# A blockwise delta-rule attention: the inverse is spread by VectorE, its rows are placed whole, and the block gather moves one chunk ahead

## The reference

```python
k_n = k / (np.linalg.norm(k, axis=-1, keepdims=True) + 1e-06)
for t in range(S):
    y[:, :, t] = einsum('bhd,bhde->bhe', q[:, :, t], state)
    v_old = einsum('bhde,bhd->bhe', state, k_n[:, :, t])
    state = state + beta_t * einsum('bhd,bhe->bhde', k_n[:, :, t], v_t - v_old)
```

## Time and profile before

| What | Value |
|---|---|
| Median of 3 runs | 909.26 us (906.07 to 910.19) |
| The profiled execution, its own time | 906.9 us |
| Its span, first to last instruction | 905.0 us |
| PE matmul busy | 808.8 us (89%) |
| DVE busy | 510.0 us (56%) |
| ACT busy | 340.2 us (38%) |
| POOL busy | 163.8 us (18%) |
| End of PE's last attention product | 313.58 us |
| First operation of `dense` on DVE | 317.95 us |

### The profile page before, as it was taken

The page is one execution under the profiler, slowest core; times in us unless marked ns, Lnnn a source line. Parts: engine busy times, 40 slices in busy tenths (PEclk is TensorE's granted clock), DMA queues, the critical chain, the costliest instruction groups (busy, mean ns, idle before and its releaser), DMA issues.

```text
span 905.0 us, 24872 instructions
## 1 busy us (share of the span) xinstructions
PE 808.8 (89%) x10976; PEld 571.8 (63%) x10976; DVE 510.0 (56%) x1212; ACT 340.2 (38%) x659; POOL 163.8 (18%) x195
## 2 busy tenths in 40 slices
PE   5487777888877689999999999999999999999998
PEld 4487777788877635566566656665656666666664
DVE  5666656676665157554336333636454776767522
ACT  3365555555554314322222122414233343433311
POOL 6131323132120001030003001001221332323200
PEclk9998999888999879999999999999999999999999
DMA  8022432231110022301000100000000000000001
GB/s 192 18 74 72 122 73 57 73 74 56 55 39 21 30 74 92 105 1 36 18 27 27 53 1 27 27 1 1 1 1 1 1 19 18 27 18 27 28 27 53
DMA packets 45048, 37.70 MB, mean 42 GB/s; under 512 B 27401, under 2 KB 39052, under 8 KB 44940
## 3 DMA queue, kind: packets, MB, share of 16 engines
q1 hardware_dynamic: 38020, 30.95, 12.3%
q10 hardware_dynamic: 6920, 5.15, 2.0%
HBM read 26.65 MB, written 4.72 MB: 35 GB/s over the span
## 4 chain that ended last, share of the span: by engine, by line
PE 80%; issue 8%; DVE 6%; ACT 4%; DMA 1%; SPq 1%; POOL 0%; DVEq 0%; ACTq 0%
PE bank L298 16%; PE bank L1033 5%; PE bank L1081 5%; PE bank L1079 5%; PE bank L1035 5%; PE bank L1080 5%; PE bank L1034 5%; PE bank L1017 3%; PE bank L1019 3%; PE bank L1018 3%; PE bank L330 3%; PE bank L967 2%; PE bank L353 2%; DVE hT_lo L1451 2%; PE bank L973 2%
## 5 line engine op out<-in xcount | busy, mean ns | idle before, releaser
L1199 ACT ACTIVATE hT_hi<-bank 128x384 f16<-128x384 f32 x96 | 46.8, 489 | 160.9 <-PE bank L1019 160.8
L1033 PE MATMUL bank<-wA,hT_hi 128*128 128x384 f16 x288 | 94.0, 326 | 2.8 <-DVE hT_lo L1451 2.8
L1451 DVE SCALAR_TENSOR_TENSOR hT_lo<-bank,hT_hi 128x384 f16<-128x384 f32 x96 | 53.2, 555 | 73.6 <-ACT hT_hi L1199 73.4
L1017 PE MATMUL bank<-unT,wA 128*128 128x384 f16 x288 | 93.9, 326 | 0.3 <-DVE hT_lo L1451 0.3
L1019 PE MATMUL bank<-unT,wA 128*128 128x384 f16 x288 | 93.9, 326 | 0.0
L1018 PE MATMUL bank<-unT,wA 128*128 128x384 f16 x288 | 93.9, 326 | 0.0
L1035 PE MATMUL bank<-wA,hT_lo 128*128 128x384 f16 x288 | 93.9, 326 | 0.0
L1034 PE MATMUL bank<-wA,hT_hi 128*128 128x384 f16 x288 | 93.9, 326 | 0.0
L298 PE MATMUL bank<-TT,AP 64*64 64x64 f32 x768 | 40.4, 281 | 55.3 <-issue 55.3
L298 PE MATMUL bank<-Yv,ET 64*64 64x48 f32 x2304 | 74.3, 218 | 4.6 <-ACT Yv L436 2.4
L298 PEld LDWEIGHTS bank<-Yv,ET 64*64 64x64 f32 x2304 | 72.1, 135 | 7.2 <-ACT Yv L436 4.6
(11 more groups left out here) (200 smaller groups left out, 1703.8 us busy)
## 6 DMA issues: line engine op xcount, KB each, us to landing
Kb<-k_dram SPq DMA_DIRECT2D x24, 192.0 KB, 3.4
Vv<-v_dram SPq DMA_DIRECT2D x12, 384.0 KB, 3.4
z_first<-w_dram SPq DMA_DIRECT2D x8, 576.0 KB, 3.9
z_first<-wt_dram SPq DMA_DIRECT2D x8, 576.0 KB, 3.7
out_dram<-hT_hi SPq DMA_DIRECT2D x24, 192.0 KB, 1.8
KQ<-q_dram SPq DMA_DIRECT2D x44, 96.0 KB, 2.3
X<-Yo ACTq DMA_DIRECT2D x12, 192.0 KB
X<-Yo ACTq DMA_DIRECT2D x10, 189.0 KB
```

What stands on the lines that cost most here:

```text
L1017: pe.matmul(out, w1[0][:, k, cols], unT[0][:, k, :], start=(k == 0), stop=False)
L1033: pe.matmul(out, hT[0][:, f, cols], w2[0][:, f, :], start=(f == 0), stop=False)
L1199: act.activation(hT[0][:, f, :], bank[3 + m % 3][:, 0:TG * P], ACT.Relu).then_inc(s_hh, 1)
L1451: dve.scalar_tensor_tensor(hT[1][:, f, :], bank[3 + m % 3][:, 0:TG * P], 0.0, hT[0][:, f, :], ALU.max, ALU.subtract).then_inc(s_hl, 1)
```

## The change

1. **Spread by DVE.** `scaled_u` no longer writes Us. Two `scalar_tensor_tensor` operations multiply the inverse by a row mask and by beta over the norm, and write both halves of Ux. ACT's `spread`, the tensor Us and the semaphore `s_sp` are gone.
2. **Layout.** Dy is now [P, BLK, NG, 2] instead of [P, BLK, 2, NG], and To is [P, NG, 2, BLK] instead of [P, BLK, 2, NG]. So the gather (ACT's and DVE's half) writes every second element, the transpose in `blocks_out` writes in steps of 16 elements, and `placed` reads rows of 32 contiguous elements instead of elements 32 apart. The row masks move with it, so that the choice of halves into Rb becomes one addition of two slices instead of two masked operations; IN falls from 6 to 5.
3. **Order on DVE.** `make_x` comes ahead of both `mask_e`; `blocks_out(c + 1)` follows `scaled_u(c + 1)` at once, ahead of `norm` or `scale`; and `blocks_in` is called for c+2 at the end of the turn instead of for c+1 before the elimination.
4. **Order on PE.** `predicted(c)` comes ahead of both corners, `grow(c)` ahead of both `direct`.
5. **Order on ACT.** `placed(c + 1)` comes right after `grown(c)`, ahead of both `output` copies, and `root` after them.

The block of SP is untouched by the diff: every load waits on the same count of the same semaphore as before.

```diff
@@ attention, tensors
-        Dy = sb("Dy", [P, BLK, 2, NG])
+        Dy = sb("Dy", [P, BLK, NG, 2])
-        To = sb("To", [P, BLK, 2, NG])
+        To = sb("To", [P, NG, 2, BLK])
-        Us = sb("Us", [P, BLK, BLK])
@@ PE, turn c
             for c in range(C0, NC):
+                predicted(c)
                 corner(c, 0)
-                predicted(c)
                 corner(c, 1)
...
                 out = queried(c)
+                grow(c)
                 direct(c, 0, out)
-                grow(c)
                 direct(c, 1, out)
@@ ACT
-                    copy(Dy[:, :, x, :], Ab[:, n % RA, :, BLK * x:BLK * (x + 1)].rearrange("p g j -> p j g"),
-                         scale=rows[:, 5:6]).then_inc(s_hb, 1)
-            def spread(n):
-                act.wait_ge(s_us, n + 1)
-                for x in range(2):
-                    copy(Ux[:, :, x, :], Us[:], scale=rows[:, 3 + x:4 + x]).then_inc(s_sp, 1)
+                    copy(Dy[:, :, :, x], Ab[:, n % RA, :, BLK * x:BLK * (x + 1)].rearrange("p g j -> p j g"),
+                         scale=rows[:, 5 + x:6 + x]).then_inc(s_hb, 1)
...
-                    copy(TT[:, :, 2 * BLK * y:2 * BLK * (y + 1)].rearrange("p g (x i) -> p g x i", x=2),
-                         To[:].rearrange("p i x g -> p g x i"), scale=rows[:, 5 + y:6 + y]).then_inc(s_tt, 1)
+                    copy(TT[:, :, 2 * BLK * y:2 * BLK * (y + 1)], To[:].rearrange("p g x i -> p g (x i)"),
+                         scale=rows[:, 9 + y:10 + y]).then_inc(s_tt, 1)
@@ ACT, turn c
                 copied_y(c, 3)
+                grown(c)
+                placed(c + 1)
+                output(c, 0)
+                output(c, 1)
                 if c % 2:
                     root((c + 3) // 2)
-                grown(c)
-                spread(c + 1)
-                output(c, 0)
-                placed(c + 1)
-                output(c, 1)
                 store(c)
@@ DVE, blocks_in, scaled_u, blocks_out
-                dve.tensor_scalar(Rb[:], Tt[:, :, 0, :], rows[:, 3:4], None, ALU.mult).then_inc(s_in, 1)
+                dve.tensor_tensor(Rb[:], Tt[:, :, 0, :], Tt[:, :, 1, :], ALU.add).then_inc(s_in, 1)
                 dve.wait_ge(s_in, at + 4)
-                dve.scalar_tensor_tensor(Rb[:], Tt[:, :, 1, :], rows[:, 4:5], Rb[:], ALU.mult, ALU.add).then_inc(s_in, 1)
+                dve.tensor_tensor(Ti[:], Rb[:], by, ALU.mult).then_inc(s_in, 1)
                 dve.wait_ge(s_in, at + 5)
-                dve.tensor_tensor(Ti[:], Rb[:], by, ALU.mult).then_inc(s_in, 1)
-                dve.wait_ge(s_in, at + 6)
...
-                dve.tensor_tensor(Us[:].rearrange("p i k -> p k i"), U[:], by, ALU.mult).then_inc(s_us, 1)
+                for x in range(2):
+                    dve.scalar_tensor_tensor(Ux[:, :, x, :].rearrange("p i k -> p k i"), U[:], rows[:, 3 + x:4 + x], by, ALU.mult,
+                                             ALU.mult).then_inc(s_us, 1)
...
-                dve.transpose(To[:].rearrange("p i x g -> p (i x g)"), Ux[:].rearrange("p i x k -> p (i x k)")).then_inc(s_to, 1)
+                dve.transpose(To[:].rearrange("p g x i -> p i (g x)"), Ux[:].rearrange("p i x k -> p (i x k)")).then_inc(s_to, 1)
@@ DVE, turn c
             for c in range(C0, NC):
+                make_x(c)
                 mask_e(c, 0)
-                make_x(c)
                 mask_e(c, 1)
-                blocks_in(c + 1)
-                eliminate(c + 1, (1, 2, 3, 4, 5, 6, 7))
-                if c < 0 and c % 2 == 0:
-                    scale((c + 2) // 2)
-                eliminate(c + 1, (8, 9, 10, 11, 12, 13, 14))
+                eliminate(c + 1, (1, 2, 3, 4, 5, 6, 7, 8, 9, 10, 11, 12, 13, 14))
                 scaled_u(c + 1)
+                blocks_out(c + 1)
                 if c % 2:
                     norm((c + 3) // 2)
-                elif c >= 0:
+                else:
                     scale((c + 2) // 2)
-                blocks_out(c + 1)
+                blocks_in(c + 2)
```

More of the change, by code:

```diff
@@ L68, in constants @@
     mU = np.broadcast_to(upper.reshape(1, BLK * BLK), (P, BLK * BLK))
-    z = (p // BLK) % 4
-    rows = np.concatenate([t[:, None] // BLK == np.arange(3)[None, :], z[:, None] % 2 == np.arange(2)[None, :],
-                           z[:, None] // 2 == np.arange(2)[None, :]], 1)
+    x, y, odd = (p // BLK) % 2, (p // (2 * BLK)) % 2, p % 2
+    rows = np.concatenate([t[:, None] // BLK == np.arange(3)[None, :], odd[:, None] == np.arange(2)[None, :],
+                           (2 * y + x)[:, None] == np.arange(4)[None, :], y[:, None] == np.arange(2)[None, :]], 1)
     return {
@@ L116, in attention @@
         mU = sb("mU", [P, BLK * BLK])
-        rows = sb("rows", [P, 7])
+        rows = sb("rows", [P, 11])
         bt = sb("bt", [P, NC * NG])
@@ L120, in attention @@
         ms = sb("ms", [P, 2, 2 * NG])
-        cd = sb("cd", [P, 2, 2, NG])
+        cd = sb("cd", [P, 2, NG, 2])
         cx = sb("cx", [P, 2, 2, BLK])
@@ L135, in attention @@
         s_in, s_iv = sem("block_steps"), sem("inverse_steps")
[L136 to L137 removed]
+        s_hb, s_us, s_to, s_tt = sem("upper_blocks"), sem("inverse_scaled"), sem("inverse_turned"), sem("TT_made")
         s_e, s_et = sem("E_product"), sem("E_masked")
@@ L204, in attention @@
         STEPS = 2 + 28
-        IN = 6
+        IN = 5
         NS = 11
@@ L574, in scale @@
                 if pair >= 2:
-                    dve.wait_ge(s_us, 2 * pair - 2)
+                    dve.wait_ge(s_us, 2 * (2 * pair - 2))
                 m = ms[:, pair % 2, :]
-                both = [P, 2, 2, NG]
+                both = [P, 2, NG, 2]
                 steps = [
@@ L586, in scale @@
                     lambda: dve.tensor_tensor(
-                        cd[:], nr[:, 5, :].rearrange("p (n g) -> p n g", n=2).unsqueeze(2).broadcast_to(both),
-                        bt[:, 2 * pair * NG:2 * (pair + 1) * NG].rearrange("p (n g) -> p n g", n=2).unsqueeze(2).broadcast_to(both),
+                        cd[:], nr[:, 5, :].rearrange("p (n g) -> p n g", n=2).unsqueeze(3).broadcast_to(both),
+                        bt[:, 2 * pair * NG:2 * (pair + 1) * NG].rearrange("p (n g) -> p n g", n=2).unsqueeze(3).broadcast_to(both),
                         ALU.mult),
-                    lambda: dve.transpose(cx[:].rearrange("p n x i -> p (n x i)"), cd[:].rearrange("p n x g -> p (n x g)")),
+                    lambda: dve.transpose(cx[:].rearrange("p n x i -> p (n x i)"), cd[:].rearrange("p n g x -> p (n g x)")),
                     lambda: dve.tensor_scalar(cT[:, pair % 2], cx[:, :, 0, :], rows[:, 3:4], None, ALU.mult),
@@ L605, in blocks_in @@
                     dve.wait_ge(s_hb, 2 * n + x + 1)
-                    dve.scalar_tensor_tensor(Dy[:, :, x, :],
+                    dve.scalar_tensor_tensor(Dy[:, :, :, x],
                                              Ab[:, n % RA, :, BLK * (x + 2):BLK * (x + 3)].rearrange("p g j -> p j g"),
-                                             rows[:, 6:7], Dy[:, :, x, :], ALU.mult, ALU.add).then_inc(s_in, 1)
+                                             rows[:, 7 + x:8 + x], Dy[:, :, :, x], ALU.mult, ALU.add).then_inc(s_in, 1)
                 dve.wait_ge(s_in, at + 2)
-                dve.transpose(Tt[:].rearrange("p j x i -> p (j x i)"), Dy[:].rearrange("p j x g -> p (j x g)")).then_inc(s_in, 1)
+                dve.transpose(Tt[:].rearrange("p j x i -> p (j x i)"), Dy[:].rearrange("p j g x -> p (j g x)")).then_inc(s_in, 1)
                 dve.wait_ge(s_in, at + 3)
@@ L651, in blocks_out @@
                     return
-                dve.wait_ge(s_sp, 2 * n + 2)
+                dve.wait_ge(s_us, 2 * n + 2)
                 if n:
                     dve.wait_ge(s_tt, 2 * n)
-                dve.transpose(To[:].rearrange("p i x g -> p (i x g)"), Ux[:].rearrange("p i x k -> p (i x k)")).then_inc(s_to, 1)
+                dve.transpose(To[:].rearrange("p g x i -> p i (g x)"), Ux[:].rearrange("p i x k -> p i (x k)")).then_inc(s_to, 1)
             def mask_e(n, u):
```

8 lines of the change are left out of this document (2 added, 6 removed).

## The result

The changed kernel takes 865.61 us (median of 4, 862.92 to 867.78) against 908.61 for the kernel before: a ratio of 0.9528 (95% interval 0.9491 to 0.9564), 43 us off. Forecast were 853 us and a range of 845 to 870. The time lies in the range. The direction and the stage were right; the gain is 14 us smaller than the sum of 57.1 behind the forecast.

What follows compares the result with a forecast made beforehand. PE waiting for the inverse before each corner, then running at a low clock, was taken as the bound; 43.0 + 13.6 + 3.0 - 1.0 - 1.5 = 57.1 us off gave 852.2, plus 1 for DVE: 853 us, range 845 to 870.

Steps and rivals of the forecast that it cites:

- the sum of 57.1: Whole kernel: 43.0 pauses, 13.6 fronts and 3.0 opening saved, less 1.0 for Dy writes and 1.5 for exposed pauses, in us.
- Which stage, which chain: Attention stage: PE waits for the inverse before corners, through DVE and ACT's blocked queue; 43.0 us of pauses fall away.
- PE-bound as summed: Attention turns: PE's work sets the turn, 18.2 us; 846 to 858 us, chance 0.60.
- the rival in which DVE is the bound: Attention turns: DVE's work, lengthened beside POOL, sets the turn; 857 to 869 us, chance 0.23.
- The path of the inverse: Each attention turn, solve to TT: To ready at 9.9 us, TT at 15.1, so the corner waits for nothing.
- 1 us had been set aside for it: ACT's copies into Dy: writing in steps of two costs 0.1 us a turn, 1 us in all.
- The opening: Before the first solve: fewer operations and reordering start it at about 36.9 instead of 40.28, about 3 us saved.
- The clock: Fronts (corner, predicted, corner): the low clock follows PE's pause; without it 3.35 us instead of 4.59, 13.6 us saved.
- DVE nearly as long as PE: Attention turns: DVE's mean turn becomes 18.0 to 18.7 us against PE's 18.2; 1 us added to the forecast.
- a quarter more time exposed makes 1.5: Attention stretches, about 6 us over plain turns: PE's mid-product pauses can also fall where waits were, costing 1.5 us.
- a rival cause of the long pauses: Pauses before corners: PE's supply of instructions, not the inverse, causes them; 909 us less 3, chance 0.03.

Runs made afterwards that it cites:

- e4_warm: The kernel before, with 14 products of 128x128 of the identity added on PE at the end of every turn; 899.53 us, 0.9921 of the kernel before.
- e3_dve: The changed kernel with two spare 128x512 transposes on DVE at the end of every turn; 865.97 us, 0.9544 of the kernel before.
- e1_wide: The changed kernel with predicted, queried and grow each issued as 4 products of 384 columns instead of 32 of 48; 832.91 us, 0.9164 of the kernel before.
- e6_pe: The changed kernel with PE's old order: first corner ahead of predicted, grow between the direct products; 867.29 us, 0.9554 of the kernel before.
- e2_light: The changed kernel with loads of K, Q and V past the first rings fetching one group only; 862.07 us, 0.9505 of the kernel before.
- e5_gather: The changed kernel with the gather put back: blocks_in(c+1) ahead of the elimination; 861.53 us, 0.9516 of the kernel before.
- e7_act: The changed kernel with ACT's old order: root ahead of grown, placed between the two outputs; 866.94 us, 0.9567 of the kernel before.
- e8_both: The changed kernel with blocks_in(c+1) back ahead of the elimination and blocks_out behind norm or scale; 864.15 us, 0.9519 of the kernel before.
- e10_tiny: The changed kernel with 32 more products of one column in predicted; 888.54 us, 0.9816 of the kernel before.
- e9_diag: The changed kernel with ET block-diagonal, a hop issuing 16 products of 128x128 instead of 32 of 64x64; 992.97 us, 1.0934 of the kernel before.

## Why the prediction was right, and where its sum was off

- *Which stage, which chain.* Right. Eleven pauses for the inverse are gone, and with them the slow clock of the fronts behind them; that is where the gain comes from. After the last product the two kernels differ by 1 us. The last product ends at 272.60 us, not at about 257, and the turns last 20.2 to 21.0 us and not 18.2 to 18.6.
- *The range.* Partly luck. PE-bound as summed was to give 846 to 858, and 865.6 lies outside that. It lies in the 857 to 869 of the rival in which DVE is the bound, and this rival's mechanism did not occur.
- *The path of the inverse.* Right in nearly each piece. To starts 8.7 us after the solve and is complete at 9.8 (9.5 to 9.9 said), TT's copies take 0.721 us (0.7 said), the transposed write 1.078 against 0.709, at the upper bound of 0.35 more. ACT's Dy copies take 0.752 against 0.738, so writing in steps of two is nearly free; 1 us had been set aside for it, 0.3 was due. DVE's scaled operations take 0.666, not 0.594, and lie under cover.
- *The opening.* 3 us said, 2.9 measured, but not piece by piece. The single addition into Rb took 1.00 us beside POOL's work, and Ti now took 1.58 instead of 0.83, so the steps from Rb to Ti lasted 2.6 us instead of 3.3: 0.7 saved and not 1.5. TT was complete at 33.3 and not 32.5. The first solve waited for `make_x`, as said, and so this cost only 0.4 us (37.34 against 36.9).
- *The clock.* Right, and confirmed by e4_warm: without a pause the front runs at 1.00. The 13.6 us set for it were low. PE's busy time fell by 16.0. PE is busy for 3.02 us in the front of chunk 7 (179.30 to 183.35) where 3.35 was reckoned, and for 2.94 in e4_warm. Part of the difference is in the rows that it was priced by: the corner's was at the lower clock level until 110.84, for its first 0.11 us, and the 1.11 us taken for `predicted` includes the end of its last matmul, which overlaps the next product (start to start, `predicted` takes 0.99 us, 179.30 to 180.29).
- *DVE nearly as long as PE.* Wrong as a danger. Rb, Ti and the mask took 0.43 us each on average in their new place, without the collisions with POOL that Ti had before (the earlier trace rows against the earlier trace rows); DVE is busy for 15.09 to 16.19 us of a turn, and e3_dve adds to it for nothing. The 1 us added for it was not due, and the rival with 862 us as its middle is refuted, although the time came out beside it. The Trainium skill, "SBUF — State Buffer", section "SBUF: two separate sides", says that a GpSimd operation that reads SBUF and a DVE operation with two SBUF inputs exclude each other. In the opening of the changed kernel the trace agrees (Ti 1.58 us at 20.43 beside POOL's work), and so it does at 52 to 55 us (Ti 0.93, the mask 1.59); from 70 us on the two never met, and Rb, Ti and the mask took 0.42 to 0.43 us each time.
- *The step that failed* is the term for PE's pauses without a releaser: "a quarter more time exposed makes 1.5". It was mis-sized: the waits for a block grew by 21.2 us, from 7.4 to 28.6. PE's time without work fell by 22.0 us, where 43.0 less 1.5 and less the 0.3 due for Dy would be 41.2: 19.2 short. The pauses in the stretches before had been read as rare disturbances of 6 us in all. They are waits for the next block of 256 instructions, and each long wait for TT had let the supply catch up. With the long waits gone, it takes back about 1 us in two or three places of each turn. The prediction did name PE's supply of instructions, but only as a rival cause of the long pauses (0.03), for which it was rightly refused; it was not carried over to what would be left once they were gone. The rest runs the other way: 2.4 us more from PE's busy time, 1.5 from `dense`, 0.7 not needed for Dy; and 0.4 lost in the last transfers.
- In sum: 57.1 - 19.2 + 2.4 + 1.5 + 0.7 - 0.4 = 42.1, which is what lies between the spans.

What is shown: the pauses stand only at one place of a block of 256 of PE's records, and end 1.2 to 1.7 us after an instruction packet does (all 31 of the changed kernel); they shrink with fewer instructions (e1_wide) and when PE waits for something else (e6_pe); and they hardly depend on the amount of data loaded (e2_light), on DVE's load (e3_dve), or on the order of ACT's and DVE's work (e5_gather, e7_act, e8_both). The profile itself names no releaser for them; this is read from the times of the packets. e10_tiny, meant to add instructions without work, added work. What sets the pace of the supply stays open: no two packets of this stage start less than 3.3 us apart in any run, and no run shows why.

## What to carry to other kernels

When a wait of several us per loop turn is removed, ask what it was hiding for the engine that waited, its own instruction stream included: count its instructions per turn and look for pauses without a releaser in the middle of its products. Whether they are waits for instructions can be tested in one trace: see whether the number of PE's records before each has the same remainder by 256, and whether each ends at the same distance from an instruction packet. Price the clock together with the pause: here the front after a 4 us pause cost 1.6 us more. Once one limit sets the turn, several orders are equally good, so a change of many parts need not owe its gain to all of them.

## What the runs showed of the hardware

- PE pausing about 1 us for its next block of instructions, two or three times in 20 us, at some 1300 instructions a turn. Each such pause stands at the same place of a block of 256 records and ends 1.2 to 1.7 us after a 16 KB packet on queue 8; in the attention stage these packets start 3.3 us apart or more in every run, 4.04 on average in the changed kernel. With 25% fewer instructions a quarter of the pauses was left (28.6 to 6.9 us).
- 128x128 fp32 matmuls of 48 columns at 118 ns each at the full clock, pairs of 64x64 ones at 62 ns for the same work; and one-column products on four tiles that cost nearly as much as those of 48 columns (0.9 against 1.0 us for 32 calls).
- A granted clock of 0.77 in a turn where PE was busy for 98% of the time (e9_diag), so a falling clock is no proof of idle time.
